# The last tile's second layer held feature-major for six of its seven products

## What is computed

```python
attn = linear attention with decay, per head (B=4, H=8, S=768, D=64)
x = attn.transpose(0, 2, 1, 3).reshape(3072, 512)

h = np.maximum(x @ w_in, 0.0)              # first layer, d_ff 2048
x = h * h @ w_out

rms = np.sqrt(np.mean(x * x, axis=-1, keepdims=True) + 1e-06)
xn = x / rms * rms_g                       # second layer, d_ff 1536
g = xn @ w_gate
out = (g * (1.0 / (1.0 + np.exp(-g))) * (xn @ w_val)) @ w_out
```

## Time and profile before

| what | us |
| --- | --- |
| median of 3 runs | 1065.9 |
| lowest and highest run | 1065.86 and 1066.55 |
| the profiled execution | 1065.99 |
| its span in the trace | 1064.2 |
| TensorE busy in the span | 1056.0 |
| VectorE, ScalarE, GpSimd busy | 877.6, 610.3, 332.7 |
| the last back run, from its first matmul to the end of the span | 63.4 |

### The profile page before, as it was taken

The page is one execution under the profiler, slowest core; times in us unless marked ns, Lnnn a source line. Parts: engine busy times, 40 slices in busy tenths (PEclk is TensorE's granted clock), DMA queues, the critical chain, the costliest instruction groups (busy, mean ns, idle before and its releaser), DMA issues.

```text
span 1064.2 us, 15678 instructions
## 1 busy us (share of the span) xinstructions
PE 1056.0 (99%) x5974; PEld 884.6 (83%) x5974; DVE 877.6 (82%) x940; ACT 610.3 (57%) x887; POOL 332.7 (31%) x244
## 2 busy tenths in 40 slices
PE   8999999999999999999999999999999999999998
PEld 7887788888888888888888888888888888888898
DVE  5896989878779878789899988978886986978684
ACT  4765775557664666654674645656454555544353
POOL 1864550004540015430034554005444102544000
PEclk9999999999999999999999999999999999999999
DMA  9999568664438644365642335632225751130455
GB/s 357 402 412 418 216 228 268 216 198 139 178 121 275 216 141 160 139 257 196 222 142 95 119 119 221 214 119 80 60 78 151 266 191 47 55 103 21 142 187 186
DMA packets 80553, 195.69 MB, mean 184 GB/s; under 512 B 24280, under 2 KB 34520, under 8 KB 75616
## 3 DMA queue, kind: packets, MB, share of 16 engines
q1 hardware_dynamic: 78016, 189.96, 51.4%
q10 hardware_dynamic: 2464, 4.74, 1.2%
HBM read 152.11 MB, written 42.48 MB: 183 GB/s over the span
## 4 chain that ended last, share of the span: by engine, by line
PE 93%; DMA 3%; POOL 1%; DVE 1%; ACT 1%; issue 0%; SPq 0%; ACTq 0%; POOLq 0%; DVEq 0%
PE Y L862 13%; PE Y L864 13%; PE Y L863 13%; PE Z L864 8%; PE Z L862 8%; PE Z L863 8%; PE X L864 8%; PE X L863 8%; PE X L862 8%; DMA item_scratch<-ops 2%; DMA raw_w<-w_b 1%; PE Z L813 1%; POOL ops L748 1%; PE X L785 1%; PE Y L785 1%; PE R L836 1%
## 5 line engine op out<-in xcount | busy, mean ns | idle before, releaser
L706 POOL TENSOR_TENSOR w_ops<-raw_w,w_ops 128x512 fp32r<-128x512 f32 x90 | 128.6, 1429 | 500.5 <-ACT w_ops L976 500.4
L1038 ACT CAST ops<-hid 128x1024 fp32r<-128x1024 f32 x147 | 154.7, 1053 | 162.8 <-PE Z L864 55.1
L1433 DVE TENSOR_TENSOR ops<-hid,ops 128x1024 fp32r<-128x1024 f32 x147 | 180.2, 1227 | 45.3 <-ACT ops L1038 44.8
L706 POOL TENSOR_TENSOR w_ops<-sums_w,w_ops 128x512 fp32r<-128x512 f32 x120 | 166.8, 1393 | 118.2 <-ACT w_ops L976 117.7
L862 PE MATMUL Y<-ops,w_ops 128*128 128x512 f32 x360 | 140.6, 391 | 0.5 <-ACT Y L1045 0.4
L864 PE MATMUL Y<-ops,w_ops 128*128 128x512 f32 x360 | 140.1, 389 | 0.0
L863 PE MATMUL Y<-ops,w_ops 128*128 128x512 f32 x360 | 140.1, 389 | 0.0
L1074 ACT ACTIVATE gt<-gt 128x512 f32<-128x512 f32 x72 | 45.1, 633 | 111.6 <-DVE gt L1650 38.9
L862 PE MATMUL Y<-ops 128*128 128x512 f32 (+1 forms) x288 | 104.5, 363 | 0.0
L863 PE MATMUL Y<-ops 128*128 128x512 f32 (+1 forms) x288 | 104.4, 362 | 0.0
L864 PE MATMUL Y<-ops 128*128 128x512 f32 (+1 forms) x288 | 104.4, 362 | 0.0
(11 more groups left out here) (180 smaller groups left out, 2320.3 us busy)
## 6 DMA issues: line engine op xcount, KB each, us to landing
ops<-item_scratch SPq DMA_DIRECT2D x147, 512.0 KB, 3.7
raw_w<-w_f SPq DMA_DIRECT2D x30, 1024.0 KB, 5.0
item_scratch<-hid SPq DMA_DIRECT2D x30, 512.0 KB, 3.1
qk_sb<-qkv SPq DMA_DIRECT2D x23, 512.0 KB, 8.6
kv_sb<-qkv SPq DMA_DIRECT2D x20, 512.0 KB, 9.5
y_scratch<-hid SPq DMA_DIRECT2D x12, 512.0 KB, 5.6
raw<-y_scratch SPq DMA_DIRECT2D x3, 2048.0 KB, 9.6
raw<-w_b SPq DMA_DIRECT2D x5, 1024.0 KB, 4.9
```

What stands on the lines that cost most here:

```text
L706: nc.gpsimd.tensor_tensor(w_ops[:, k, 1], front_w_source(m, k), f32(w_ops[:, k, 0]), ALU.subtract).then_inc(w_lo, 1)
L1038: nc.scalar.copy(hop_at(n)[:, 0], hid[:, 2 * g:2 * g + 2, OPERAND[k], :]).then_inc(hop_hi, 1)
L1433: nc.vector.tensor_tensor(hop[:, 1], hid[:, 2 * g:2 * g + 2, OPERAND[k], :], f32(hop[:, 0]), ALU.subtract).then_inc(hop_lo, 1)
```

## The change

The last tile's back run (now `last`) becomes feature-major for its products k = 0 to 5, the groups 0 to 17, as in the other tiles. Product 6 (groups 18 to 20) stays by token. What follows from that:

- The quarters A, Dd and Bb are copied or added plainly from PSUM, then turned and scaled by VectorE (`turn`, `scale_turned`, now through the idle place `last_flat` in `raw`), at n = 14, 16 and 18.
- The sum in Y that product 6 is added to (for C) is feature-major by then. ScalarE copies it to `u3` at n = 15, after VectorE has read Y; TensorE turns it back into Y with eight transposes against an identity matrix (`turn_u3`), ahead of group 18. Then product 6 is added by token, and group 20 ends the kernel as before.
- The stores of A, Dd and Bb are 8 DMAs each, of 64 KB in runs of 64 numbers, in the place of 2 each of 256 KB (`store_last_turned`). SyncE issues them, but for four of Bb's, which ScalarE issues ahead of its scaling of C.
- The hop of group 20 gets a place of its own in `ops` (`own_place`) and is made at n = 13.
- Five small DMAs are added early in the last tile's front runs: `rinv_turn` for this tile and the identity.

```diff
+    def own_place(self, n):
+        return self.last and n == self.groups - 1
...
         def hop_at(bk, n):
+            return ops[:, 0 if bk.own_place(n) else 4 + n % HR, :, :, :]
...
+            def store_last_turned(i, halves):
+                sp.wait_ge(turn_scaled, 4 * (TILES - 1) + i + 1)
+                for h, a in product(halves, range(4)):
+                    dst, src = last_turned(i, h, a)
+                    sp.dma_start(dst, src).then_inc(out_stored, 16)
...
-                load_items(bk, 8, 17)
-                if bk.by_token:
-                    store_out(t, 0)
-                load_items(bk, 17, 20)
-                if bk.by_token:
-                    store_out(t, 1)
+                load_items(bk, 8, 18)
+                if bk.last:
+                    store_last_turned(0, (0, 1))
+                load_items(bk, 18, 20)
+                if bk.last:
+                    store_last_turned(1, (0, 1))
                 load_items(bk, 20, 21)
-                if bk.by_token:
-                    store_out(t, 2)
-            store_out(TILES - 1, 3)
+                if bk.last:
+                    store_last_turned(2, (0,))
+            store_last()
...
+            def turn_u3():
+                pe.wait_ge(identity_loaded, 16)
+                pe.wait_ge(u3_saved, 1)
+                for tb, j in product(range(4), range(2)):
+                    nc.tensor.matmul(tokens(Y)[:, tb, P * j:P * j + P], u3[:, j, P * tb:P * tb + P], identity_sb,
+                                     start=(tb % 2 == 0 and j == 0), stop=True, is_transpose=True,
+                                     skip_group_check=True)
...
+                    by_token = bk.last and k == 6
                     if g == 0:
                         banks_free(bk.run, k)
-                    pe.wait_ge(hop_lo, bk.base + n + 1)
+                    if g == 0 and by_token:
+                        turn_u3()
+                    if bk.own_place(n):
+                        pe.wait_ge(own_lo, 1)
+                    else:
+                        pe.wait_ge(hop_lo, bk.base + n + 1)
                     pe.wait_ge(item_loaded[bk.w_slot(n)], 16 * bk.w_count(n))
...
                 elif t == TILES - 1:
+                    act.wait_ge(turn_scaled, 4 * t + 3)
+                    for a in range(4):
+                        dst, src = last_turned(2, 1, a)
+                        act.dma_start(dst, src).then_inc(out_stored, 16)
+                    act.wait_ge(rinv_t_loaded[t], 128)
                     for i, tb in enumerate(LAST_BLOCKS):
                         act.wait_ge(last_done, i + 1)
...
+                    if n == 5 * ng and bk.last:
+                        act.wait_ge(c22_done, run + 1)
+                        nc.scalar.copy(u3, Y[:]).then_inc(u3_saved, 1)
...
+                    if n == 4 * ng + 1 and bk.last:
+                        low_hop(bk, bk.groups - 1)
+                    if n == 4 * ng + 2 and bk.last:
+                        turn(t, 0)
+                        scale_turned(t, 0)
...
+                    if bk.last and n in (5 * ng + 1, 6 * ng):
+                        turn(t, 1 if n < 6 * ng else 2)
+                        scale_turned(t, 1 if n < 6 * ng else 2)
```

More of the change, by code:

```diff
@@ L72, in __init__ @@
         self.t, self.second = t, second
-        self.by_token = second and t == TILES - 1
+        self.last = second and t == TILES - 1
         self.run = run_b2(t) if second else run_b1(t)
@@ L428, in x_place, with last_turned @@
             return 2, b % 2, (b // 2) * 2 * P + (c - 4) * P
+        def last_turned(i, h, a):
+            m, n = divmod((A, Dd, Bb)[i], 2)
+            row = S * (n + 2 * h) + N
+            cols = slice(2 * P * m + 64 * a, 2 * P * m + 64 * a + 64)
+            place = out_sb[32 * a:32 * a + 32, (A, Dd, Bb)[i]].rearrange("j t d -> j (t d)")[:, N * h:N * h + N]
+            rows = out[row:row + S - N, cols].rearrange("(b j) d -> j b d", j=32)
+            return rows, place.rearrange("j (b d) -> j b d", d=64)
         block = ctx.enter_context(nc.Block())
@@ L559, in store_y, with store_last @@
                 sp.dma_start(y_dram[t, :, s], y_out(s)).then_inc(y_stored[s], 16)
[L561 to L580, removed]
+            def store_last():
+                m, n = divmod(C, 2)
+                for i, tb in enumerate(LAST_BLOCKS):
+                    row = CH * (n + 2 * (tb // 2)) + 4 + tb % 2
+                    sp.wait_ge(last_scaled, i + 1)
+                    sp.dma_start(out_v[:, row, m, :], out_sb[:, C, tb, :]).then_inc(out_stored, 16)
             def store_turned(t, i):
@@ L609, in spread_rinv, with spread_last_turn, load_identity @@
                         sp.dma_start(rinv_turn[rows, t], rinv_r[:]).then_inc(rinv_t_loaded[t], 16)
+            def spread_last_turn():
+                sp.wait_ge(turn_scaled, 4)
+                for i in range(4):
+                    sp.dma_start(rinv_turn[32 * i:32 * i + 32, 0], rinv_r[:]).then_inc(rinv_t_loaded[TILES - 1], 16)
+            def load_identity():
+                sp.wait_ge(front_lo, 7 * 2 * TILES)
+                sp.dma_start(identity_sb, identity).then_inc(identity_loaded, 16)
             def load_rinv_b(t):
@@ L902, in back_run @@
                     k, g = divmod(n, bk.ng)
+                    by_token = bk.last and k == 6
                     if g == 0:
                         banks_free(bk.run, k)
-                    pe.wait_ge(hop_lo, bk.base + n + 1)
+                    if g == 0 and by_token:
[4 more added lines that the diff above has]
+                        pe.wait_ge(hop_lo, bk.base + n + 1)
                     pe.wait_ge(item_loaded[bk.w_slot(n)], 16 * bk.w_count(n))
-                    hop, slot = hop_at(n), wb_at(bk.w_slot(n))
+                    hop, slot = hop_at(bk, n), wb_at(bk.w_slot(n))
                     dst = (X, Z, Y, X, Y, Z, Y)[k]
-                    if bk.second and bk.t == TILES - 1 and n == bk.groups - 1:
+                    if bk.own_place(n):
                         for i, tb in enumerate(LAST_BLOCKS):
@@ L930, in back_run @@
                                 mm = three(place, hop[:, 0, q, rows], hop[:, 1, q, rows], slot[:, 0, q, :],
-                                           slot[:, 1, q, :], first and tb % 2 == 0)
+                                           slot[:, 1, q, :], False)
                     mm.then_inc(group_done, 1)
@@ L1045, in seed, with save_p5 @@
                 nc.scalar.copy(Y[:], X[:]).then_inc(seeded, 1)
[L1047 to L1053, removed]
+            def save_p5(run):
                 act.wait_ge(*done(run, 1))
@@ L1056, in save_p5, with save_u2 @@
                     act.wait_ge(folded, 2 * TILES)
[L1057 to L1062, removed]
+                nc.scalar.copy(p5[:], Z[:]).then_inc(p5_saved, 1)
+            def save_u2(run):
                 act.wait_ge(*done(run, 2))
[L1064 to L1067, removed]
+                nc.scalar.copy(u2[:], Y[:]).then_inc(u2_saved, 1)
             def silu(run, i):
@@ L1219, in back_run @@
                 for n in range(bk.groups):
-                    if (3 if bk.second else 0) <= n < bk.groups - 2:
+                    if (3 if bk.second else 0) <= n < bk.groups - 2 and not bk.own_place(n + 2):
                         high_hop(bk, n + 2)
+                    if n == 4 * ng + 1 and bk.last:
+                        high_hop(bk, bk.groups - 1)
                     if n == bk.groups - 1 and TILES <= bk.next_front < 2 * TILES:
@@ L1247, in back_run @@
                                 act.wait_ge(out_stored, 256 * t)
[L1248 to L1256, removed]
+                            nc.scalar.copy(out_sb[:, A].rearrange("p t d -> p (t d)"),
+                                           X[:].rearrange("p z n -> p (z n)")).then_inc(x_taken, 1)
                         else:
```

84 lines of the change are left out of this document (42 added, 42 removed).

## The result

| | before | after |
| --- | --- | --- |
| median, us | 1065.86 (7 runs) | 1069.19 (7 runs) |
| lowest and highest, us | 1065.55 and 1067.38 | 1067.92 and 1072.04 |
| profiled execution: span, us | 1064.2 | 1066.7 |
| TensorE busy, us | 1056.0 | 1055.5 |

The changed kernel is slower: ratio 1.003, 95% interval 1.002 to 1.004, or 3.3 us. Forecast were 1066.9 us and a range up to 1068.8. The direction was right, but the step was 3.3 us in the place of 1.0, and the time lies outside the range. A second set of 11 runs on another occasion gave 1068.74, ratio 1.0027 (1.0019 to 1.0036): 1.8 us above the forecast, and just inside the range.

What follows compares the result with a forecast made beforehand. TensorE bounds the kernel before; with the change, group 20 waits for item 20 and starts at 1059.4 in the place of 1058.39, the tail unchanged: 1065.9 + 1.0 gives 1066.9 us, range 1065.0 to 1068.8.

Steps and rivals of the forecast that it cites:

- TensorE's gain: Last back run: 18 feature-major groups at 2.72 us each in the place of 2.88 by token, saving 2.9 us.
- The transposes: Eight transposes on TensorE ahead of group 18 take 1.0 us, with bounds of 0.5 and 2.2.
- The wait that takes its place: Before group 20, TensorE waits for item 20, issued behind the stores of A and Dd; group 20 starts 1.0 us later.
- step 5: SyncE issues Dd's eight stores from 1051.9 at 0.47 us each, 3.8 us in all, until 1055.7.
- step 6: Item 20 is issued after Dd's stores and lands 3.7 us later, so group 20 starts at 1059.4.
- From there to the end nothing changes: From group 20's start to the kernel's end: 5.8 us for four blocks, a scaling and the last store, as before.
- Edits at nothing: Parts priced at zero, among them items 18 and 19: group 18 perhaps 0.5 us late, hidden as group 20 waits.
- TensorE stays the bound: Item 20 arrives in time and the end comes 1.9 us sooner, 1064.0; chance 0.1, with cases partly between.
- The stores hold SyncE longer: Dd's stores issue at 0.73 us each or item 20 lands in 5.8: 1068.9 to 1069.1, 1071 with both; chance 0.15.
- The change doesn't bring the faster groups: Last back run's groups stay at 2.88 us, so the steps slide by 2.4 us: 1069.4; chance 0.03.
- The rule weighed: Skill page calls DMA issue time usually small; forecast instead took 3.8 us of issue against 2.5 of transfer for eight stores.

Runs made afterwards that it cites:

- e4_items_first_u3_later: Changed kernel with items 18 and 19 loaded ahead of A's stores, item 20 ahead of Dd's, and ScalarE's copy to u3 behind the cast for group 18: 1064.13 us, ratio 0.9982.
- e3_before_item_late: Kernel before the change, with item 20 loaded behind the two stores of Bb in the place of ahead of them: 1071.17 us, ratio 1.0046.
- e2_filler: Changed kernel with ten unused matmuls of 512 columns ahead of group 20's wait for its item: 1068.41 us, ratio 1.0020.
- e6_change_u3_later: Changed kernel with only ScalarE's copy to u3 one place later, SyncE's order as in the change: 1065.82 us, ratio 0.9994.
- e5_items_first_bb_on_sp: As e1_items_first, but SyncE issues all eight stores of Bb and ScalarE none: 1066.59 us, ratio 1.0007.
- e1_items_first: Changed kernel with SyncE's order alone altered, items 18 and 19 ahead of A's stores and item 20 ahead of Dd's: 1065.80 us, ratio 0.9999.
- a2_again: The changed kernel once more, unaltered, for a second trace and its spread: 1068.74 us, ratio 1.0027.

## Why the prediction was wrong, point by point

**TensorE's gain** held: 2.72 us a group over 18 groups, and e4_items_first_u3_later ran at it without a gap.

**The transposes** held: 1.0 us taken, 1.04 measured.

**The wait that takes its place** was named rightly, with its cause, its releaser and its place. By distance from the back run's first matmul: VectorE's scaling of Dd ended at 51.14 (foretold 51.1); item 20 was issued at 55.23 (54.9), since eight stores took 4.03 us and not 3.8; TensorE went on 4.0 after that (3.7 foretold). Group 20 started at 59.24 in the place of 58.6. The terms of step 5 and step 6 were short by 0.3 us each, and the late start was 1.65 us in the place of 1.0.

**"From there to the end nothing changes"** is the step that failed. I took the tail of 5.8 us over from a kernel whose TensorE never paused, while I forecast a pause of 2 to 3 us ahead of it, and no row of the trace before showed what a pause does to the granted clock. It fell to half in the first trace, and by the mean clocks in 13 executions of 18. Group 20, all of it on the path, took 4.6 in the place of 3.2 us from its start to its last block's scaling, and the tail 7.3 us in the place of 5.8. e3_before_item_late shows this price apart from the change, 1.5 to 1.6 us, and e2_filler that the fall goes with the pause. The range had no case for it: a tail longer than 5.8 us was named among the signs of being wrong, but only for late stores or ScalarE's issues. With 1.65 us for the start and 1.0 to 1.4 for the clock the sum is 1068.6 to 1069.0, against a median of 1069.2 for the thirteen executions with the fall. Without it the sum is 1067.6, against 1068.15 for the five at full clock. So 0.2 to 0.6 us stay unexplained; the start of the back run, which varies by 1.4 us between the traces, could hold them, but that is not shown.

**"Edits at nothing"** held: the wait before group 18 was 0.81 us, 0.5 foretold, and lay under that for item 20. In e6_change_u3_later, with that cover gone, it is 1.2 us and is paid.

**The rivals.** *TensorE stays the bound*, 1064.0, was rightly ruled out for this order of SyncE; with the order altered and the copy moved it came true at 1064.1, and with the order alone not (1065.8), since ScalarE's issues stopped TensorE. *The stores hold SyncE longer*, with 0.15, was near the measured time for another reason: it needed 1.1 us beyond steps 5 and 6, and there were 0.6; the issue pace was 0.50 us, not 0.73. *The change doesn't bring the faster groups* did not happen.

**The rule weighed.** That issuing is small against the transfer (the Trainium skill, "DMA: Bandwidth & Descriptors", "Issuing engines are not separate DMA queues") did not hold for these stores: eight took 3.9 to 4.3 us to issue in every trace, while in the changed kernel the DMA engines were busy for 0.57 of 1052 to 1057, so that the transfer is some 2.3 us of the 4.0 (an estimate from that share). The forecast's 2.5 us of transfer was given without its working; 512 KB at the 224 GB/s of the earlier trace rows make 2.3. And e5_items_first_bb_on_sp, which puts Bb's all on one engine, gained nothing over e1_items_first, though TensorE no longer waited. As to a DMA's signal behind earlier writes, no run told it apart; item 20 took 3.9 us to land, at most 0.3 above what I took.

A rule that I left out bears on the failed step. In the two traces of the changed kernel the clock fell to half after a pause of 2.44 us and stayed after one of 2.17. The Trainium skill, "TensorE: Matmul & The Clock Gate", in the table of "Why this matters for your kernels", warns against pauses between bursts of matmuls, as the clock drops back after them. The runs agree that a pause can halve the clock; the pauses that the page warns of are longer than the 2.44 us that came before the fall here, so in this case the runs decide.

## What to carry to other kernels

When a forecast contains a new pause of the engine that bounds the kernel, price what comes after the pause too: here the same matmuls ran at half clock in 13 executions of 18, at 1.0 to 1.6 us, so that taking the pause away is worth more than its length. Filling it gives back the clock's part alone. A queue that issues loads in order must not have stores ahead of them that wait for late work: moving the loads ahead of the stores was worth 2.9 us here. And an engine's wait for a result of another stops all that is behind it: a copy that is needed 3 us later belongs behind the cast that is needed at once.

## What the runs showed of the hardware

- TensorE's granted clock fell to 0.50 after single pauses of 2.44 us (in the changed kernel) and 3.47 us (e3_before_item_late), and not after 2.17 or 1.54 us (a2_again, e1_items_first), in kernels that had kept it busy for a millisecond. With a pause of 2.2 to 2.4 us it is not certain: 13 of 18 executions had a lowered mean, and with the pause filled 0 of 11. What decides it in a single execution is open.
- The fall comes late: in the changed kernel the window of the pause still shows 1.00, and the half clock begins about 0.5 us after TensorE had gone on (e3_before_item_late: 0.9). It lasted 3.4 us in both, with TensorE busy.
- A DMA of 256 runs of 256 bytes cost SyncE 0.48 to 0.54 us to issue (3.87 to 4.31 for eight) and ScalarE 0.50 to 0.65 (2.00 to 2.58 for four). In the changed kernel the DMA engines were busy for 0.57 of 1052 to 1057, so that it was the issue that set the pace.
